# Attention with the values as the stationary operand, in two halves of TensorE's columns

## The reference

```python
scores = scale * np.matmul(q, k.transpose(0, 1, 3, 2))          # 4 x 8 x 576 x 576
thresh = np.max(scores, axis=-1, keepdims=True) - tau
scores = np.where(scores >= thresh, scores, -1000000000.0)
scores = scores - np.max(scores, axis=-1, keepdims=True)
attn = np.exp(scores)
attn = attn / (np.sum(attn, axis=-1, keepdims=True) + 1e-09)
return np.matmul(attn, v).astype(np.float32)
```

## Time and profile before

| | us |
|---|---|
| median of three runs | 1158.19 |
| the profiled execution, its own time | 1158.84 |
| its span, first to last instruction | 1157.1 |
| attention (first scores matmul to the last logits) | 13.4 to 392.9 |
| the two stages behind it | from 393.2 |
| one pair of heads in the first half, 9 steps | 20.8 |

### The profile page before, as it was taken

The page is one execution under the profiler, slowest core; times in us unless marked ns, Lnnn a source line. Parts: engine busy times, 40 slices in busy tenths (PEclk is TensorE's granted clock), DMA queues, the critical chain, the costliest instruction groups (busy, mean ns, idle before and its releaser), DMA issues.

```text
span 1157.1 us, 19451 instructions
## 1 busy us (share of the span) xinstructions
PE 1107.7 (96%) x6835; PEld 1020.6 (88%) x6836; DVE 550.1 (48%) x919; ACT 506.8 (44%) x897; POOL 214.1 (19%) x187
## 2 busy tenths in 40 slices
PE   4999999999999889999999989999999999999995
PEld 4999999999999768888888879999999899999994
DVE  5777777666657656366345246322322223223221
ACT  4777777768766635355335343221221211212211
POOL 2533444442421012212211110010010100100101
PEclk9999999999989989999999999999999999999998
DMA  4222332332101336366455133010010010100000
GB/s 165 98 76 85 135 104 79 113 138 68 56 1 63 113 111 243 129 208 234 138 190 191 38 102 112 26 55 1 1 55 1 22 35 1 55 1 1 28 1 28
DMA packets 34276, 95.47 MB, mean 83 GB/s; under 512 B 2888, under 2 KB 5192, under 8 KB 34192
## 3 DMA queue, kind: packets, MB, share of 16 engines
q1 hardware_dynamic: 28112, 73.05, 18.4%
q0 software_dynamic: 5904, 21.26, 5.4%
q10 hardware_dynamic: 176, 0.02, 0.0%
HBM read 79.36 MB, written 14.95 MB: 82 GB/s over the span
## 4 chain that ended last, share of the span: by engine, by line
PE 63%; DVE 1%; issue 1%; DMA 1%; POOL 0%; ACT 0%; DVEq 0%; POOLq 0%
PE hb L1105 13%; PE hp L1055 10%; PE yp L1082 10%; PE hp L1119 9%; PE gp L1105 7%; PE vp L1105 7%; PE xb L1119 4%; PE hb L1067 2%; PE xb L1040 1%; PE yp L1090 1%; DMA x_in<-x_rows,token_of 1%; POOL out L1027 0%; DVE r_row_b L1417 0%; DVE xt_lo L1336 0%; PE gp L1147 0%
## 5 line engine op out<-in xcount | busy, mean ns | idle before, releaser
L358 PE MATMUL o_ps<-v_in,prob_t 128*128 128x66 f32 (+1 forms) x1440 | 180.2, 273 | 0.0
L358 PEld LDWEIGHTS o_ps<-v_in,prob_t 128*128 128x128 f32 x1440 | 174.6, 194 | 0.0
L536 DVE TENSOR_REDUCE neg_max<-scores 128x1 f32<-128x576 f32 x144 | 108.9, 756 | 104.0 <-PE scores L321 103.7
L414 ACT ACTIVATE prob_t<-scores 128x640 f32<-128x640 f32 (+3 forms) x163 | 112.8, 692 | 92.0 <-PE scores L331 87.0
L548 DVE SCALAR_TENSOR_TENSOR prob<-scores,thresh,expo 128x576 f32<-128x576 f32 x144 | 116.5, 809 | 3.4 <-ACT expo L407 3.4
L331 PE MATMUL scores<-ident,prob 128*128 128x128 f32 x720 | 105.0, 277 | 6.7 <-DVE prob L548 6.7
L321 PE MATMUL scores<-kt_hi,qt 128*128 128x288 f32 x320 | 104.1, 341 | 6.1 <-DVE kt_lo L608 3.0
L407 ACT ACTIVATE expo<-scores,neg_max 128x576 f32<-128x576 f32 x144 | 107.1, 744 | 6.0 <-DVE neg_max L536 6.0
L1105 PE MATMUL hb<-f_xt_hi,w_hi 128*128 128x384 f32 x288 | 97.4, 338 | 0.0
L1105 PE MATMUL hb<-f_xt_hi,w_lo 128*128 128x384 f32 x288 | 96.6, 335 | 0.0
L1105 PE MATMUL hb<-f_xt_lo,w_hi 128*128 128x384 f32 x288 | 96.5, 335 | 0.0
(11 more groups left out here) (239 smaller groups left out, 2434.4 us busy)
## 6 DMA issues: line engine op xcount, KB each, us to landing
stage<-in_moe_w SPq DMA_DIRECT2D x18, 1024.0 KB, 5.3
stage_more<-in_moe_w SPq DMA_DIRECT2D x14, 1024.0 KB
q_raw<-in_q SPq DMA_DIRECT2D x16, 640.0 KB, 5.2
k_raw<-in_k SPq DMA_DIRECT2D x16, 576.0 KB, 3.8
ys<-y_out POOLq DMA_DIRECT2D x21, 256.5 KB, 3.1
v_in<-in_v SPq DMA_DIRECT2D x16, 330.0 KB, 2.9
stage<-in_moe_w_val SPq DMA_DIRECT2D x3, 1024.0 KB, 5.4
rows<-ys POOLq DMA_DIRECT2D x3, 769.5 KB, 4.6
```

Source lines behind the costliest of these rows:

```text
L358: last = nc.tensor.matmul(dst, prob_t[:, u % 3, 128 * c:128 * (c + 1)], src, start=(c == 0), stop=(c == KEY_CHUNKS - 1))
L414: nc.scalar.activation(prob_t[:, u % 3, 0:cols], scores[u % 3][:].rearrange("p a c -> p (a c)")[:, 0:cols], ACT.Copy).then_inc(s_pt_sb, 1)
L536: V.tensor_reduce(neg_max[:, t:t + 1], scores[u % 3][:, :, 0:HALF], mybir.AxisListType.XY, ALU.max, negate=True).then_inc(s_max, 1)
```

## The change

The two operands of the values' matmul trade places, and all around it follows:

- The tiles of a pair alternate between the sides (`side_of`: tile t is side t % 2), and the values' matmuls run for two tiles at once, behind tiles 1, 3, 5, 7 and 8 (`BOTH`). The values of one side (128x64) stand in one half of the array's columns, those of the other side in the other half, and each side's turned probabilities (128 columns) pass through. The program gives these matmuls a tile of 128x64 of the array at column 0 or 64; all others have 128x128.
- The result is the output turned (`o_t`, 64 features of each side by 128 rows), copied by ScalarE. A new kind of unit, `ROWS`, turns a pair's five pieces back (5 transposes, L384) and copies them to `o_sb` in four instructions (L481 to L487). It stands behind step 3 of the next pair, and takes one of the three PSUM buffers in its turn. In the last pair there are five such units with one piece each, two among the steps and three behind them.
- `prob_t` has 4 buffers in place of 3, and `prob` is gone: the mask is written over the exponential.
- The row sums are `accum_out` of the mask; the ones are gone from the values.
- `keys_scaled` moves from ScalarE to GpSimd; for pair 0 VectorE does scaling and subtraction in one.

```diff
+BOTH = (1, 3, 5, 7, 8)
+ROWS_BEHIND = 3
...
         order.append((STEP, g))
+        if p and t == ROWS_BEHIND:
+            order.append((ROWS, (p - 1, None)))
+        if p == PAIRS - 1 and t in (6, 7):
+            order.append((ROWS, (p, t - 6)))
...
+    order += [(ROWS, (PAIRS - 1, n)) for n in (2, 3)]
+    last = [(LOGITS, n) for n, (_, at) in enumerate(LOGIT_UNITS) if not at]
+    return order + last[:1] + [(ROWS, (PAIRS - 1, 4))] + last[1:]
...
+            def outputs_t(u, p, n):
+                pe.wait_ge(s_pt_sb, u - 2)
+                parts = range(5) if n is None else [n]
+                pe.wait_ge(s_o_sb, MADE[UNIT_OF[STEP, TILES * p + min(2 * parts[-1] + 1, 8)]] + 1)
...
+                    last = nc.tensor.transpose(dst[:, 128 * b:128 * (b + 1)], o_t[:, p % 2, part, :], ident[:])
...
                 for c in range(KEY_CHUNKS):
-                    if t < 8:
-                        dst, src = o_ps[u % 2][:, 0:V_COLS], v_in[:, p % 3, c, t // 4, :]
...
-                    last = nc.tensor.matmul(dst, prob_t[:, u % 3, 128 * c:128 * (c + 1)], src,
-                                            start=(c == 0), stop=(c == KEY_CHUNKS - 1))
+                    for side in range(2):
+                        src = turned(u if t == 8 or side else UNIT_OF[STEP, g - 1])
+                        last = nc.tensor.matmul(made(u)[D * side:D * (side + 1), 0:128], v_in[:, p % 3, c, side, :],
+                                                src[:, 128 * c:128 * (c + 1)], start=(c == 0), stop=(c == KEY_CHUNKS - 1))
...
-                    if what == STEP:
+                    if what == STEP and g % TILES in BOTH:
                         values(u - 2, g)
...
+            def rows_out_of(u, p):
+                act.wait_ge(s_pt, u + 1)
...
+                nc.scalar.activation(o_sb[:, p % 2, 0:4, :],
+                                     src[:, 0:MAIN].rearrange("p (i s d) -> p i s d", s=2, d=D)[:, :, 0, :], ACT.Copy)
...
-                V.scalar_tensor_tensor(prob[:, g % 3, :].rearrange("p (a c) -> p a c", a=2), scores[u % 3][:, :, 0:HALF],
-                                       thresh[:, t:t + 1], expo[:, g % 3, :].rearrange("p (a c) -> p a c", a=2),
-                                       ALU.is_ge, ALU.mult).then_inc(s_prob, 1)
+                V.scalar_tensor_tensor(probs, scores[u % 3][:, :, 0:HALF], thresh[:, t:t + 1], probs, ALU.is_ge, ALU.mult,
+                                       accum_out=row_sum[:, p % 2, col:col + 1]).then_inc(s_prob, 1)
...
-                pool.wait_ge(s_k_scaled, p + 1)
+                pool.wait_ge(s_k_hi, p + 1)
+                nc.gpsimd.tensor_scalar(k_raw[:, par, :], k_raw[:, par, :], k_scale[:], None, ALU.mult).then_inc(s_k_scaled, 1)
```

More of the change, by code:

```diff
@@ L234, in attention, with turned, made, values_made @@
         block = ctx.enter_context(nc.Block())
+        def turned(u):
+            return prob_t[:, TURNED[u] % 4, :]
+        def made(u):
+            return o_ps[MADE[u] % 2]
+        user = {}
+        for u in TURNED:
+            what, g = UNITS[u]
+            user[TURNED[u]] = UNIT_OF[STEP, g + 1] if what == STEP and g % TILES not in BOTH else u
+        def values_made(p):
+            return MADE[UNIT_OF[STEP, TILES * p + 8]] + 1
+        def rows_out(p, n=None):
+            return UNIT_OF[ROWS, (p, n)] + 1
         def k_ready(p):
@@ L419, in values_out @@
                 p, t = g // TILES, g % TILES
-                act.wait_ge(s_o, u + 1)
-                if p >= 2 and t == 0:
-                    act.wait_ge(s_x, p - 1)
-                if t < 8:
-                    last = nc.scalar.activation(o_sb[:, p % 2, row_tile(t), :], o_ps[u % 2][:, 0:V_COLS], ACT.Copy)
-                else:
-                    for side in range(2):
-                        rows = slice(TAIL * side, TAIL * (side + 1))
-                        last = nc.scalar.activation(o_sb[rows, p % 2, row_tile(t), :],
-                                                    o_ps[u % 2][rows, V_COLS * side:V_COLS * (side + 1)], ACT.Copy)
@@ new lines, in last_rows_out @@
+            def last_rows_out(u, n):
+                act.wait_ge(s_pt, u + 1)
+                act.wait_ge(s_last_inv, 2 * n + 2)
+                src, cols = scores[u % 3][:].rearrange("p a c -> p (a c)"), slice(FEAT - D, FEAT)
+                for side in range(2):
+                    rows = slice(0, 128) if n < 4 else slice(TAIL * side, TAIL * (side + 1))
+                    t = 8 if n == 4 else 2 * n + side
+                    last = nc.scalar.activation(x_sb[rows, TILES + row_tile(t), cols], src[rows, D * side:D * (side + 1)],
+                                                ACT.Copy, scale=row_inv[rows, 1, t:t + 1])
+                last.then_inc(s_pt_sb, 1)
@@ L491, in _ @@
             keys_hi(0)
-            keys_scaled(0)
             act.wait_ge(s_warm, 2)
@@ L501, in _ @@
                         transposed_out(u, KEY_CHUNKS * 128)
+                    elif what == ROWS and g[1] is None:
+                        rows_out_of(u, g[0])
+                    elif what == ROWS:
+                        last_rows_out(u, g[1])
                     else:
@@ L612, in _ @@
             max_tile(0, 0)
-            for u in range(behind(STEPS - 1) + 2):
+            for u in range(behind(STEPS - 1)):
                 what, g = UNITS[u + 1]
```

177 lines of the change are left out of this document (83 added, 94 removed).

## The result

The changed kernel takes 1198.36 us (median of 4 runs, 1197.88 to 1200.45) and the kernel before, timed beside it, 1157.20. The ratio is 1.0355, with an interval of 1.0318 to 1.0392: slower by 41 us. The forecast was 1202.

What follows compares the result with a forecast made beforehand. TensorE looked like the bound, with ScalarE's copy 0.14 us behind as the floor of 2.15 a step. 15 pairs at +2.8 (+41), +4 for the end, about 1 back: +44 on 1158.84, by the median 1202 us; range 1183 to 1282.

Steps and rivals of the forecast that it cites:

- The floor: Attention steps without values: transposes, ScalarE's copy out of PSUM, then scores take 2.15 us; only a middle over 0.95 lengthens them.
- Halves at once: Values' passes in both column halves of the array run concurrently: 1.1 us a group; 50% with a small switching cost.
- Change of form: Switching the array into and out of halves around each values group: 0.085 us, twice a group, giving steps of 2.42.
- full stop: Rival: array drains at each switch around values groups, 0.27 us each time, +30 us, 1232; chance 20%.
- A pair: One pair of heads in attention: 5 x 2.15 + 5 x 2.42 + 0.53 + 0.2 = 23.6 us, before 20.82.
- The sum: Whole kernel: 41 + 4 = 45, about 1 back, so +44 us; stages behind attention as long as before.
- the end: Last pair's outputs turned back in five units, two inside and three behind the last tile: +4 us, bounds 1 to 7.
- TensorE alone as the pace: Rival: TensorE's work bounds attention, a pair takes 16.9 us, 1096 in all; not slower 8%, of which 3% faster.
- Halves in turn: Rival: values' two column halves never overlap, 2.2 us a group, +88 us less a few hidden, 1285; chance 15%.
- The clock: Rival: TensorE's clock falls four to ten times more, 3 to 5 us each, 1220 to 1250; chance 7%.
- At no cost: Edits forecast at nothing: keys scaled on GpSimd, 1.1 to 2.6 us but hidden; accumulator read 0.07 a step on VectorE.
- The second loop: Transposes, copy, scores, VectorE's maximum, threshold and mask, transposes two units on: 2.05 us a step, 2.08 with accumulator, under 2.15.

Runs made afterwards that it cites:

- the in-turn order: Changed kernel with all values matmuls of one side queued ahead of the other side's, same matmuls and sums; 1250.92 us, ratio to before 1.0801.
- the run with the whole array: Changed kernel with both sides' values as one 128-column stationary, 10 passes instead of 20, one tile's product left out; 1206.66 us, 1.0420 (attention 423.1).
- the one with the old form: Kernel before the change, with the copy out of PSUM in two; 1146.28 us, ratio 0.9885.
- the run without ready sums: Changed kernel with the mask's accumulator output removed and the row sums constants, output not normalised; 1200.05 us, ratio 1.0372.

## Why the prediction was right

*The floor.* Right: 2.14 to 2.18 us without values (forecast 2.15), from a row of before in which the middle was short. Cutting the copy in two gives 31 of the 47 us back, and doing without the tenth step gives 32; the two overlap with the change of form, so these amounts don't add up to 47.

*Halves at once.* Right: 20 passes 0.057 us apart in the mean (1.15 us; predicted 1.1), shown against the in-turn order. The Trainium skill, "TensorE: Matmul & The Clock Gate", Part 3, has column groups running concurrently, and the trace agrees, with pass starts 0.007 us apart in each pair.

*Change of form.* The term that was too small. A step with values is 2.51 for the forecast 2.42 (0.64 + 1.24 + 0.63 for 0.54 + 1.1 + 0.61 and twice 0.085). Against the run with the whole array the edges cost 0.14 going in and 0.19 coming out, 0.16 each way in the mean, where I took 0.085 from the change of type. That lies a hair outside the 0 to 0.15 of the case that I had called the likeliest, about midway to the full stop of 0.27. The Trainium skill, "TensorEngine Tiling (Array Packing)", Key Properties, has a change of mode drain the engine. The trace agrees that a change costs something, but at 0.14 and 0.19 it is below the full stop that I priced at 0.27 each way. On either edge the next pass starts 0.20 us behind a pass that the profile models as 0.27 long, so whether the array is empty in between isn't shown.

*A pair.* Predicted 23.6, measured 23.78. Step by step: five steps with values are 2.51 or 2.52, one of them 2.57, for 2.42, +0.54; ScalarE's four copies, forecast at +0.2, cost nothing, since the step of turning back holds values too and is 2.51 anyway (they appear as soon as it is shorter, in the whole-array run), -0.2; one step of 2.00 for 2.15, which has no scores of its own and waits for the mask, -0.15. So errors of either sign nearly cancel: that the pair came out within 0.2 is partly luck.

*The sum.* Attention ends 47.1 us later, predicted 44. To the first transpose of the last pair of heads it is 39.9 us (404.66 for 364.74), and the last pair with its tail takes 35.7 for 28.5, 7.1 more. One pair's 2.96 taken off, 4.2 are left for the end, forecast at 4 (1 to 7). Between pair and pair it is less even than the sum had it: those with logits take -0.3 to +4.8 us more, 2.2 in the mean and not 2.96, and the first pair, which has no step of turning back and for which I had forecast nothing, takes 2.4 more. The stages behind took 5.3 us less than before, predicted none. So the total is made of two misses of opposite sign, +3 in attention and -5 behind it.

The 5.3 us aren't the change's: in the ten other kernels (the whole-array one apart, the one with the old form among them) these stages took 758.2 to 760.7 us, and 763.9 in the profiled execution of before. Its trace shows where it lost them. TensorE's clock fell at 412 us, when its work began again behind a wait, and at 914 behind another wait. From its chain, two groups of 24 matmuls at the fallen clock and later, then the wait and the matmuls behind it:

```profile
413.40 8.35 PE hp L1055 x24
424.05 5.75 PE hp L1055 x24
910.56 1.82 issue
912.38 2.98 PE gp L1105 x12
915.36 3.05 PE vp L1105 x12
```

After's chain has 5.73 for the first of these groups, no wait in front of `gp`, and 2.10 and 2.08 for the last two. That is 2.6 us at the first place and 1.8 + 0.9 + 1.0 = 3.7 at the second, less 1.0 that before was ahead elsewhere: 5.3. Whether the other executions of before lose the same, no trace shows.

*The rivals.* TensorE alone as the pace (1096) is ruled out: the mean step is (23.78 - 0.53) / 10 = 2.3 against the 2.01 that it needed, and TensorE is idle for 18% of the first window. Full stop: ruled out at its price, by 0.14 and 0.19 against 0.27. Halves in turn: ruled out, and mis-sized. The clock: in attention TensorE's clock fell four times (at 59, 288, 335 and 359 us, 3.4 us each) and a fifth time for its last 2.6 us (granted clock 0.51 from 437.7 to 440.3), where before it fell once (at 327, 6.8 us). The window in which it falls first, and the one ahead:

```profile
52.00:59.00 7.00, 5.41 (x51) 4.60 (x50) 5.11 (x12) 4.76 (x11) 6.12 (x3) 0.99 0.13 34
59.00:66.00 7.00, 6.21 (x46) 5.46 (x46) 3.41 (x8) 2.96 (x6) 4.15 (x2) 0.77 0.37 147
```

TensorE had been busy for 5.41 of 7 us, and ran at half clock for about half of the next 7. That pair of heads took 25.34 us for the plain 23.78 (and 23.77 in the run without ready sums, where the clock didn't fall there), so this fall cost 1.6 us, not the 3 to 5 that I took. The rival's additional falls came, at about half their price or less: 3 to 5 of the 47 us, net of the fall before, an estimate from this one fall. My sum had not allowed for them.

*At no cost.* The pass on GpSimd took 3.20 us, outside my bounds of 1.1 to 2.6, and it is hidden, as said. The accumulator's cost is nothing: shown.

*The second loop.* I put it at 2.08 a step. No run shows it as a bound: without the accumulator nothing moved, and with the copy in two, which would take it to 1.83, the gain ended at another wait for the mask, at 2.00, behind scores that were late for TensorE's own values. The prediction didn't have that wait.

## What to carry to other kernels

Before taking work off the busiest engine, look for a step in which that work happens to be short and read how long the step is: if it is as long as the others, the work was cover for a wait, and removing it buys nothing. A new step in such a chain costs the whole chain once more, however little it holds, so small work should be put in an existing step's empty middle. Cutting the hand-over in two (here the copy and the wait on its first part) shortens the chain itself; after it, look at once for the next wait (here the mask's, 2.00 us a step where 1.5 was hoped for).

## What the hardware showed that I had not expected

- Two column halves overlap even when they are queued one after the other: the second half's first pass starts 0.32 us before the first half's last, 1.85 us for 20 passes, where 1.15 is the alternating order and 2.2 would be no overlap.
- Going into the halves on a warm array costs 0.14 us and coming out 0.19, each less than the 0.27 that the profile models for a single pass.
- The passes of 64 stationary and 128 moving columns come in pairs every 0.109 us, so two tiles' values take what one tile's took before (0.112 from start to start with 66 moving columns, 0.113 with 132).
- GpSimd multiplies 128x1152 float32 by a scalar of each partition in 3.20 us, 0.56 longer than it takes to subtract two such tensors.
